# Attention, expert layer and feed-forward in one kernel: expert outputs stored in the experts' order, half of them transposed under the last item, output scattered

## What is computed

```python
B, H, S, D = 4, 12, 448, 64          # attention
q_n, k_n = rmsnorm(q, g_q), rmsnorm(k, g_k)
x = softmax(q_n @ k_n.T / sqrt(D)) @ v          # then rows (b, s), columns (h, d): 1792 x 768

# expert layer: 8 experts, one for each token
xn, en = x / (norm(x) + 1e-6), emb / (norm(emb) + 1e-6)
logits = xn @ en.T / tau
e = argmax(logits)                               # expert of a token
gate = softmax(logits)[e]
y[mask_e] = gate * (relu(x[mask_e] @ w1[e]) @ w2[e])      # 768 -> 1024 -> 768

h = y @ w_in                                     # feed-forward: 768 -> 2048 -> 768
out = max(0.01 * h, h) @ w_out
```

## Time and profile before

| | |
|---|---|
| Median of 3 runs | 1268.63 us (1266.11 to 1270.06) |
| The profiled execution | 1267.65 us, span of its instructions 1265.9 us |
| PE busy | 1204.3 us (95%) |
| DVE busy | 876.1 us (69%) |
| ACT busy | 736.6 us (58%) |
| POOL busy | 540.3 us (43%) |
| Mean granted clock of TensorE | 0.978 |

### The profile page before, as it was taken

The page is one execution under the profiler, slowest core; times in us unless marked ns, Lnnn a source line. Parts: engine busy times, 40 slices in busy tenths (PEclk is TensorE's granted clock), DMA queues, the critical chain, the costliest instruction groups (busy, mean ns, idle before and its releaser), DMA issues. The chain is left out here.

```text
span 1265.9 us, 21116 instructions
## 1 busy us (share of the span) xinstructions
PE 1204.3 (95%) x6986; PEld 1065.1 (84%) x6986; DVE 876.1 (69%) x1156; ACT 736.6 (58%) x1386; POOL 540.3 (43%) x592
## 2 busy tenths in 40 slices
PE   4999999999579999999999968999999999999998
PEld 3888888888459999999999857999999999999997
DVE  4999999999669999999999953555322245551222
ACT  5999999999628788888888724222321122221111
POOL 7998888886456676767666630000000000000000
PEclk9999999999779999999999987999999999999999
DMA  2244343321134555655551023121322312201132
GB/s 70 60 132 123 97 110 99 87 74 45 37 113 187 188 204 214 223 208 202 217 212 61 13 83 104 50 59 59 92 72 74 90 56 78 74 32 56 52 88 74
DMA packets 102027, 131.95 MB, mean 104 GB/s; under 512 B 28824, under 2 KB 81304, under 8 KB 101920
## 3 DMA queue, kind: packets, MB, share of 16 engines
q1 hardware_dynamic: 94464, 108.58, 27.8%
q0 software_dynamic: 3360, 16.52, 3.6%
q10 hardware_dynamic: 4096, 5.51, 1.3%
HBM read 193.09 MB, written 19.27 MB: 168 GB/s over the span
## 5 line engine op out<-in xcount | busy, mean ns | idle before, releaser
L880 ACT CAST w_hi<-w_raw 128x768 fp32r<-128x768 f32 (+1 forms) x294 | 250.5, 931 | 17.0 <-DMA w_raw<-moe_w_in 7.2
L1058 DVE TENSOR_TENSOR w_lo<-w_raw,w_hi 128x1024 fp32r<-128x1024 f32 x82 | 182.4, 2260 | 1.4 <-ACT w_hi L880 1.3
L1466 DVE TENSOR_TENSOR out_lo<-out_raw,out_hi 128x384 fp32r<-128x384 f32 x64 | 35.7, 558 | 170.9 <-ACT out_hi L1375 170.9
L742 POOL TENSOR_TENSOR w_lo<-w_raw,w_hi 128x1024 fp32r<-128x1024 f32 x44 | 111.2, 2531 | 96.8 <-ACT w_hi L880 96.7
L1257 PE MATMUL ps_acc<-yT_hi,in_hi 128*128 128x448 f32 x384 | 142.1, 370 | 2.1 <-DVE yT_lo L1452 2.1
L1287 PE MATMUL ps_acc<-gT_hi,out_hi 128*128 128x448 f32 x384 | 142.8, 372 | 0.0
L1258 PE MATMUL ps_acc<-yT_hi,in_lo 128*128 128x448 f32 x384 | 141.1, 367 | 0.0
L1259 PE MATMUL ps_acc<-yT_lo,in_hi 128*128 128x448 f32 x384 | 140.9, 367 | 0.0
L1289 PE MATMUL ps_acc<-gT_lo,out_hi 128*128 128x448 f32 x384 | 140.7, 366 | 0.0
L1288 PE MATMUL ps_acc<-gT_hi,out_lo 128*128 128x448 f32 x384 | 140.6, 366 | 0.0
L1369 ACT ACTIVATE small_h<-ps_acc 128x448 f32<-128x448 f32 x64 | 34.8, 544 | 179.7 <-PE ps_acc L1259 179.7
(11 more groups left out here) (194 smaller groups left out, 2881.5 us busy)
## 6 DMA issues: line engine op xcount, KB each, us to landing
w_raw<-moe_w_in SPq DMA_DIRECT2D x80, 1536.0 KB
in_raw<-moe_w_in_in SPq DMA_DIRECT2D x32, 384.0 KB, 3.3
out_raw<-moe_w_out_in SPq DMA_DIRECT2D x64, 192.0 KB, 2.4
qk_raw<-q_in SPq DMA_DIRECT2D x48, 112.0 KB, 2.0
qk_raw<-k_in SPq DMA_DIRECT2D x48, 112.0 KB, 2.1
v_raw<-v_in SPq DMA_DIRECT2D x48, 112.0 KB, 2.0
x_rows<-x_tok SPq DMA_DIRECT2D x48, 112.0 KB, 2.5
in_raw<-x_rows SPq DMA_DIRECT2D x16, 336.0 KB, 3.3
```

The lines of the kernel that those rows point to most:

```text
L880: act.copy(out[:, c, :], raw[:, c, :]).then_inc(s_hi, 1)
L1058: dve.tensor_tensor(w1_lo[:, c, :], w1_raw[:, c, :], w1_hi[:, c, :].bitcast(F32), ALU.subtract).then_inc(s_w1lo, 1)
```

## The change

1. `x_rows` has the tokens in natural order and 8 more columns: the logits of a token stand behind its x, stored by SP with one more DMA for each batch. The gather brings both.
2. The gate is worked out item by item, for the slots in their order. ScalarE squares the gathered rows in every item, GpSimd does power, add, power and multiply (`exponent`), VectorE the maximum of the logits (`top`), ScalarE the exponents and their sum (`exp`), GpSimd add and power (`gate_of`). The ReLU has the gate as its scale. `gate_exponents`, `gates`, `gate_y` and the 16 loads of x are gone.
3. `slot_rows` is the rank of a token in the order of the experts (`ranks` on VectorE, 16 more small products on PE, `ranks_of_slots`), so that the first 896 rows of `y_rows` are complete after 14 items. A 769th column of y holds the token's number.
4. SP loads the first seven tiles of 128 rows of y under the last item. PE transposes three ahead of the last product2 and one after each of its chunks 3 to 6. ScalarE and VectorE split them into `w1_hi` and `w1_lo`, which the feed-forward keeps, and the first block of w_in too.
5. The feed-forward has 14 tiles of 128 rows and starts with its products. Its 28 results are scattered by GpSimd (indirect DMA with `out_index`, made of the token's number), no longer stored by ScalarE.

The diff, cut to its core:

```diff
@@ attention, SP
-    x_dest = x_rows.rearrange("(p t b) d -> p t (b d)", t=T, b=B)
+    x_dest = x_rows.rearrange("(b p t) d -> p t b d", t=T, b=B)
...
+                if h == H - 1:
+                    sp.wait_ge(s_lg, b + 1)
+                    sp.dma_start(x_dest[:, :, b, H * D:H * D + E], rt["logits"][:, :, :].rearrange("p (t b) e -> p t b e", t=T)[:, :, b, :]).then_inc(s_x_out, 16)
@@ experts, SP
+            def load_tile(j):
+                if j == 0:
+                    for u in range(2):
+                        sp.wait_ge(s_y_out[u], uses(READY - 1 - (READY - 1 - u) % 2, u))
...
+                sp.dma_start(y_tile[j], y_rows[j * P:(j + 1) * P, :]).then_inc(s_yg[j], 16)
-            for u in range(2):
-                sp.wait_ge(s_y_out[u], uses(items - 1 - (items - 1 - u) % 2, u))
@@ experts, GpSimd
+                pool.tensor_copy(y_sb[u][:, DM:DM + 1], slot_in[:, n:n + 1]).then_inc(s_id, 1)
+                pool.wait_ge(s_id, n + 1)
...
+            def exponent(n):
+                pool.wait_ge(s_xss, n + 1)
+                pool.tensor_tensor(one(x_norm, n), one(x_ss, n), consts["half"][:, 0:1], ALU.pow).then_inc(s_norm, 1)
+                pool.wait_ge(s_norm, n + 1)
+                pool.tensor_tensor(one(x_more, n), one(x_norm, n), eps_f[:, :], ALU.add).then_inc(s_more, 1)
+                pool.wait_ge(s_more, n + 1)
+                pool.tensor_tensor(one(x_inv, n), one(x_more, n), ones_f[:, :], ALU.pow).then_inc(s_inv, 1)
+                pool.wait_ge(s_inv, n + 1)
+                pool.wait_ge(s_top, n + 1)
+                pool.tensor_tensor(one(shift, n), one(x_inv, n), one(neg_top, n), ALU.mult).then_inc(s_shift, 1)
+
+            def gate_of(n):
+                pool.wait_ge(s_exps, n + 1)
+                pool.tensor_tensor(one(denom_more, n), one(denom, n), tiny_f[:, :], ALU.add).then_inc(s_denom, 1)
+                pool.wait_ge(s_denom, n + 1)
+                pool.tensor_tensor(one(gate, n), one(denom_more, n), ones_f[:, :], ALU.pow).then_inc(s_gate, 1)
...
             def body(n, u):
                 if n >= 2:
-                    lo2(n - 1)
+                    lo2(n - 1, pool2(n - 1)[:1])
+                gate_of(n)
+                if n >= 2:
+                    lo2(n - 1, pool2(n - 1)[1:])
                     store_y(n - 2, u)
                 if n + 2 < items:
                     gather(n + 2, u)
                 if n + 1 < items:
                     lo1(n + 1)
+                    exponent(n + 1)
...
+            for j in range(TILES):
+                index(j)
             store_y(items - 2, items % 2)
             store_y(items - 1, (items - 1) % 2)
@@ experts, PE
-            product2(items - 1, (items - 1) % 2, 0, C2)
+            for j in range(3):
+                transpose_tile(j)
+            for c in range(C2):
+                product2(items - 1, (items - 1) % 2, c, c + 1)
+                if 3 <= c < TILES:
+                    transpose_tile(c)
@@ experts, ScalarE
-                act.activation(h_sb[:, half * H1:(half + 1) * H1], ps_h[:, half, 0:H1], ACT.Relu).then_inc(s_relu, 1)
+                act.wait_ge(s_gate, n + 1)
+                act.activation(h_sb[:, half * H1:(half + 1) * H1], ps_h[:, half, 0:H1], ACT.Relu, scale=gate[:, n:n + 1]).then_inc(s_relu, 1)
...
+            def exp(n, u):
+                act.wait_ge(s_shift, n + 1)
+                act.activation(exps[u][:, :], x_g[u][:, DM:X], ACT.Exp, bias=shift[:, n:n + 1], scale=x_inv[:, n:n + 1],
+                               accum_out=denom[:, n:n + 1]).then_inc(s_exps, 1)
@@ experts, VectorE
-            gates()
             copy_y(items - 2, items % 2)
             for c in range(C2 // 2, C2):
                 lo2(items - 1, c)
+            for j in range(TILES):
+                y_lo(j)
+            in_low()
             copy_y(items - 1, (items - 1) % 2)
@@ feed_forward, GpSimd
+            def store(tile):
+                pool.wait_ge(s_o, tile + 1)
+                n_pass, j = tile // TILES, tile % TILES
+                row, dh = TILES * (n_pass // 2) + j, n_pass % 2
+                pool.indirect_dma_start(out=out_halves, out_offset=bass.IndirectOffsetOnAxis(ap=out_index[:, row, dh:dh + 1], axis=0),
+                                        in_=out_buffers[out_slot(tile)], in_offset=None).then_inc(s_store[out_slot(tile)], 16)
```

More of the change, by code:

```diff
@@ L582, in experts @@
     H1, H2 = F // 2, DM // 2
-    R, T, B = gate.shape
-    J = T * B
+    R, J, _ = rt["logits"].shape
+    N = R * J
+    T = 4
+    X = DM + E
+    TILES = N // P // 2
+    READY = (N // 2 - 1 + (E - 1) * (P - 1)) // P + 1
+    w1_hi, w1_lo, xT_hi, xT_lo, y_sb, out_index = (shared[k] for k in ("w1_hi", "w1_lo", "xT_hi", "xT_lo", "y_sb", "out_index"))
     items = rt["free_plus"].shape[1]
@@ L614, in experts @@
         hT_lo = [sb(f"hT_lo{u}", [P, C2, P], F32R) for u in range(2)]
-        y_sb = [sb(f"y_sb{u}", [P, DM]) for u in range(2)]
         slot_in = sb("slot_in", [P, items], I32)
@@ L790, in place @@
                 last.then_inc(s_put, 1)
+                pe.wait_ge(s_place2, 1)
+                for j in range(J):
+                    last = pe.matmul(ps_ranked, in_lane[j], in_item_ranked[:, j, :], start=j == 0, stop=j == J - 1)
+                last.then_inc(s_put2, 1)
             def transpose_x(n, u):
@@ L850, in product2, with transpose_tile @@
                     last.then_inc(s_2, 1)
+            def transpose_tile(j):
+                pe.wait_ge(s_yg[j], 16)
+                if j == 0:
+                    pe.wait_ge(s_xhi, items)
+                    pe.wait_ge(s_xlo, items)
+                    pe.wait_ge(s_relu, items * 2)
+                    pe.wait_ge(s_hhi, items)
+                    pe.wait_ge(s_hlo, items)
+                if j > 2:
+                    pe.wait_ge(s_yhi, j - 2)
+                    pe.wait_ge(s_ylo, j - 2)
+                for c in range(C1):
+                    last = pe.transpose(ps_tiles[j % 3][:, c // 3, (c % 3) * P:(c % 3 + 1) * P], y_tile[j][:, c * P:(c + 1) * P], consts["ident"][:, :])
+                last.then_inc(s_yt, 1)
             rank()
@@ L914, in body @@
                 if n >= 2:
-                    for c in range(C2):
+                    for c in range(C2 // 2):
+                        hi2(n - 1, c)
+                exp(n, u)
+                if n >= 2:
+                    for c in range(C2 // 2, C2):
                         hi2(n - 1, c)
@@ L943, in _ @@
                 hi2(items - 1, c)
+            for j in range(TILES):
+                y_hi(j)
+            in_high()
         @block.vector
@@ L1006, in rows_of_slots @@
             def rows_of_slots():
                 dve.wait_ge(s_put, 1)
-                has = ps_slot[:, 0:items]
-                dve.scalar_tensor_tensor(slot_in[:, :], has, -1.0, rt["zeros"][:, :], ALU.add, ALU.max).then_inc(s_slots, 1)
-                dve.scalar_tensor_tensor(free[:, :], has, 0.0, rt["free_plus"][:, :], ALU.is_equal, ALU.mult).then_inc(s_step, 1)
-                dve.wait_ge(s_step, 17)
-                dve.scalar_tensor_tensor(slot_rows[:, :], has, -1.0, free[:, :], ALU.add, ALU.add).then_inc(s_step, 1)
@@ L1014, in rows_of_slots, with ranks_of_slots @@
-                dve.wait_ge(s_step, 18)
+                dve.scalar_tensor_tensor(slot_in[:, :], ps_slot[:, 0:items], -1.0, rt["zeros"][:, :], ALU.add, ALU.max).then_inc(s_slots, 1)
+            def ranks_of_slots():
+                dve.wait_ge(s_put2, 1)
+                has = ps_ranked[:, 0:items]
+                dve.scalar_tensor_tensor(free[:, :], has, 0.0, rt["free_plus"][:, :], ALU.is_equal, ALU.mult).then_inc(s_free, 1)
+                dve.wait_ge(s_free, 1)
+                dve.scalar_tensor_tensor(slot_rows[:, :], has, -1.0, free[:, :], ALU.add, ALU.add).then_inc(s_ranked, 1)
@@ L1094, in _ @@
                 lo2(0, c)
+            ranks_of_slots()
             x_lo(0)
+            top(0, 0)
             for c in range(C2 // 2, C2):
@@ L1124, in _, with feed_forward @@
                 lo2(items - 1, c)
+            for j in range(TILES):
+                y_lo(j)
+            in_low()
             copy_y(items - 1, (items - 1) % 2)
-def feed_forward(nc, consts, y_rows, gate, w_in, w_out, in_raw, s_in_in, out):
+def feed_forward(nc, consts, y_rows, w_in, w_out, in_raw, s_in_in, shared, s_y_out, stored, out):
     DM, F = w_in.shape
     C, G = DM // P, F // P
-    R, T, B = gate.shape
-    J = T * B
-    TILES = J // 2
-    W = TILES * R
+    N = out.shape[0]
+    TILES = N // P // 2
+    W = TILES * P
     Q = W // 2
@@ L1296, in transpose_out @@
                 j = tile % TILES
-                pe.wait_ge(s_oT[j // T], (tile // TILES + 1) * K)
+                for half in touched(j):
+                    pe.wait_ge(s_oT[half], (tile // TILES + 1) * K)
                 if tile > 1:
```

408 lines of the change are left out of this document (207 added, 201 removed).

## The result

The changed kernel takes 1298.66 us in the median of 4 runs (1298.1 to 1300.97), the kernel before 1268.87 us (1266.11 to 1270.06) in the runs beside it: ratio 1.0241, 95% interval 1.0221 to 1.0262. It is slower by 2.4%. The profiled execution took 1300.97 us, its span is 1299.2 us (before 1267.65 and 1265.9), the granted clock 0.981 in the mean.

A forecast was written before the change was run, and what follows sets the result against it. TensorE was busy throughout the expert items, with GpSimd's and VectorE's shared way to SBUF nearly full. 1267.65 us +41 - 19.2 - 1.6 + 6 + 1 = 1294.9, as median 1296 us; forecast's own range 1273 to 1316.

The forecast's parts named there:

- Items 2 to 20, +41: Expert stage: seven small GpSimd instructions and VectorE's splits delay each other, +2.3 us in each of 18 periods (0 to +59).
- The walk: One expert item traced by "first asked, first served": waits of 6.4 to 6.8 us, about 21.2 us an item, +3.1.
- Last items and start of the feed-forward, -19.2: Expert stage's end to first hidden products: gate steps, loads and waits go, products start at 755.9 instead of 775.2 us.
- Three fill the wait of 2.10: Last items: three of the seven new tile transposes fit into PE's 2.10 us wait for y_sb.
- The 5.03 us from scatter to the next block: Expert block's end: the feed-forward's first instruction comes 5.03 us behind the last scatter.
- Feed-forward -1.6: Feed-forward: 48 y transposes become 42 and 72 output ones 63, at 0.1 us each.
- Tail +6: Kernel's end: seven GpSimd scatters at 1.3 us each replace the last stores, +6 us (+4.5 to +7.5).
- Routing +1: Routing: last logits sent after x +0.65, VectorE's small instructions 0.3; +1 us (+0.6 to +2.7 if 32-byte rows land late).
- 1, small instructions hidden: Expert stage: the small GpSimd instructions cost only +0 to +0.5 us an item, 1255 us; chance 0.26.
- 2, in between: Expert stage: +0.55 to +1.0 us an item, 1265 to 1272 us, no change to be told; chance 0.08.
- 3, the clock drops in each item: Expert stage: waits drop PE's clock, mostly covered if GpSimd paces, else +1 us an item more, 1314 to 1330; chance 0.06.
- 4, no gain at the hand-over: Feed-forward's start: PE idles 9 us and stays at clock 0.50 as before; 4 us less gain, 1300 us; no chance given.

The follow-up runs named there:

- e2: Kernel before plus seven two-input one-column GpSimd instructions an item at the change's places, on inputs made once, no other engine waiting for them: 1300.24 us, ratio 1.0242.
- e3: Kernel before plus seven one-column GpSimd memsets an item, which read nothing, at the places of e2's seven: 1273.84 us, ratio 1.0024.
- e7: Changed kernel, seven small GpSimd instructions kept but on constant columns, waits between them and other engines cut, gate's values left out: 1292.80 us, ratio 1.0179.
- e1: Changed kernel without the seven small GpSimd instructions an item; constants replace the gate's values, ScalarE copies the row number: 1258.12 us, ratio 0.9905.
- e4: Changed kernel with one small GpSimd power an item; multiply and reciprocal on VectorE, row-number copy on ScalarE, two sums dropped: 1256.64 us, ratio 0.9891.
- e5: e4 with the last copy of y out of PSUM and its scatter moved to the head of the feed-forward block: 1245.80 us, ratio 0.9814.
- e12: e4 with slot_rows allocated ahead of the stages' buffers, so those behind it lie 84 bytes further: 1254.40 us, ratio 0.9885.
- e6: e4 with the last seven output stores as plain transfers on ScalarE's queue, a quarter of the output left unwritten: 1252.13 us, ratio 0.9862.
- e10: Changed kernel with one w2 split an item moved from GpSimd to VectorE, the seven small instructions kept: 1265.83 us, ratio 0.9968.

## Why the prediction was right, and where not

**Items 2 to 20, +41: right in kind, 3 us too much.** The mechanism is the one given, GpSimd and VectorE in each other's way; e2 and e3 show it apart from the rest. The walk had five of the seven instructions waiting in every item, 4.2 us in all; in the trace it is 3.3 us, three of them in most items. Without the chain that makes 1.6 us an item (e7, e2), below the +2.3 taken. A part that the working named but gave no number fills it up: ScalarE's exponent behind GpSimd's multiply, 0.5 us an item. Two errors, of about -0.7 and +0.5, nearly cancel, and that is luck. The own time of the small instructions was right (3.0 us with gaps, 2.4 without), the choice near the walk's end too high.

**Last items and start of the feed-forward, -19.2: measured -12.6.** This is the step that failed. "Three fill the wait of 2.10" did not hold: the tiles' transposes themselves wait for hT_lo, and VectorE, with nine splits in 13.89 us, brought it 3.32 us late; the clock fell with it. Item 20's products with w1 also take 10.0 us against 8.4, with waits for VectorE's chunks in them. The working let the new load end with the 18th period, but item 20's small instructions and splits run on into the last items. The chain is not to blame: e7, without it, takes 108.2 us for this stretch, the changed kernel 105.8, e1 99.9. Only the third tile is transposed into the PSUM from which hT_lo is made, but the kernel puts the wait for it ahead of all three; whether the first two ahead of that wait would win something was not tried. With the small ones gone (e1, e4) the term is -18.5 and -18.4, so the rest of its working stood, the gap of 9 us too (8.73).

**The 5.03 us from scatter to the next block** were right as a size (796.56 to 801.65 here), and e5 shows their cause: the scatter, with the copy ahead of it. Without it the next block begins 2.0 us behind the last product.

**Feed-forward -1.6: -0.9.** Fifteen transposes fewer are of the size of what moves this stretch without any such edit (1.2 us in e2 and e3, 2.5 in e12), so the two numbers tell little.

**Tail +6: +6.2**, shown by e6, with a pitch of 1.28 us for 1.3 and 5.4 us behind the last scatter for 5.03. The Trainium skill's formula ("DMA: Bandwidth & Descriptors", section "Anatomy of one DMA — SWDGE (gpsimd) path") gave an estimate of 2.5 us from issue to landing of such a scatter; the trace has 2.6 us in the median of the 28. The 3.0 that the prediction put beside it was that of scatters twice as large. The tail still came out no shorter, since those 5.4 us are more than this landing.

**Routing +1: +2.9, outside its bound of +2.7.** Item 0 begins 1.4 us later (355.32 against 353.95), near the +1: ScalarE's first cast, behind the last logits, starts at 335.74 and not 334.81. The other 1.5 us lie in items 0 and 1, for which the working had nothing. 1.4 of them are in item 0, where the granted clock was 0.81 in the mean, before 0.86; in e10, with all seven small instructions and 0.86, item 0 takes 14.4 us instead of 15.6 (before 14.2). So most of this goes with the clock, and what set it there stays open.

**Rivals.** 1, small instructions hidden: no, +2.1 us an item, four times its threshold. 2, in between: no. 3, the clock drops in each item: no, it stays at 1.00 through the waits of at most 1.4 us. Its other half, that a fall would be mostly covered if GpSimd paces, is what e2 and e7 show. 4, no gain at the hand-over: no, but a third of it was lost for another reason. The sum for the profiled execution was 1294.9 and it took 1301.0: 6.1 us more, of which the items give -3.2, the hand-over +6.6, the routing +1.9 and the other two +0.9. That the medians lie only 2.7 us apart (1296 and 1298.7) is luck again: the profiled execution was the slowest of the four, 2.3 us above their median, where the prediction took it to be 1.0 below.

## What to carry to other kernels

Where two engines share a way and both are nearly full, count an added instruction by how often it must get in, not by its own length: seven of 0.2 to 0.5 us cost 1.6 us an item, and a gate of one such instruction with the rest as one-input instructions on VectorE and a copy on ScalarE cost nothing that can be measured (e4). Taking one large split off the fuller engine won 1.7 of the 2.1 us back (e10). A chain that hops between engines needs a price of its own, as does what the slowed engine carries past the loop's end. A block that ends with a scatter makes the next wait for it; moving that scatter and its copy across the border gave 7.8 us here.
